# Three small VectorE operations of a routing step issued earlier and without a wait behind each

## The reference, cut to what matters

```python
def reference(**kwargs):
    attn_out = _attn_ref(...)                       # 4 x 8 heads, 768 positions, windowed attention
    x = attn_out.transpose(0, 2, 1, 3).reshape(3072, 512)
    x = _moe_ref(x=x, ...)                          # layer 0: 8 experts, each row goes to one
    return _moe2_ref(x=x, ...)                      # layer 1: 8 experts again, chosen anew

def _moe2_ref(x, expert_emb, tau, w1, w2):
    xn = x / (norm(x) + 1e-06)
    en = expert_emb / (norm(expert_emb) + 1e-06)
    logits = xn @ en.T / tau
    expert_idx = argmax(logits, axis=1)             # which expert of layer 1 gets the row
    ...
    out[mask] = gate_w[mask, None] * (relu(x[mask] @ w1[e]) @ w2[e])
```

## Time and profile before

| what | value |
|---|---|
| median of 3 runs | 1096.17 us |
| profiled execution, its own time | 1095.2 us |
| span of its instructions | 1093.6 us |
| PE, busy share of the span | 94% |
| DVE, busy share | 55% |
| ACT, busy share | 31% |
| POOL, busy share | 18% |
| mean granted TensorE clock | 0.980 of full speed |
| layer 0, from the first ranks to the last | 253 to 695 us |

### The profile page before, as it was taken

The page is one execution under the profiler, slowest core; times in us unless marked ns, Lnnn a source line. Parts: engine busy times, 40 slices in busy tenths (PEclk is TensorE's granted clock), DMA queues, the critical chain, the costliest instruction groups (busy, mean ns, idle before and its releaser), DMA issues.

```text
span 1093.6 us, 24687 instructions
## 1 busy us (share of the span) xinstructions
PE 1028.2 (94%) x6898; PEld 737.1 (67%) x6898; DVE 600.8 (55%) x2649; ACT 343.2 (31%) x1125; POOL 195.9 (18%) x390
## 2 busy tenths in 40 slices
PE   5999999989989999999999998999999999999994
PEld 4788888876756657675767664776667676675772
DVE  6678888855495676566656566433343334333331
ACT  4667766734132232222222222112122112121111
POOL 1022222221131222122222112211111111111111
PEclk9999999999999999999999999999999999999997
DMA  9965557663133514151415152514615153311110
GB/s 176 214 155 138 145 135 222 261 246 113 35 103 127 187 49 174 40 185 48 175 40 187 36 189 69 178 49 151 229 39 192 40 192 113 122 32 44 39 33 19
DMA packets 123518, 134.65 MB, mean 123 GB/s; under 512 B 82220, under 2 KB 82220, under 8 KB 123312
## 3 DMA queue, kind: packets, MB, share of 16 engines
q1 hardware_dynamic: 92672, 53.06, 19.2%
q10 hardware_dynamic: 23104, 59.11, 15.0%
q0 software_dynamic: 7664, 21.56, 5.5%
HBM read 105.55 MB, written 26.92 MB: 121 GB/s over the span
## 4 chain that ended last, share of the span: by engine, by line
PE 56%; issue 23%; DMA 9%; POOL 4%; DVE 4%; POOLq 1%; ACT 1%; ACTq 1%; DVEq 0%; SPq 0%
PE bank L1520 15%; PE bank L1530 14%; PE bank L1418 9%; DMA bins<-q_in,sidx 9%; PE bank L1460 5%; PE bank L1499 4%; PE bank L1646 3%; PE bank L1625 3%; POOL q_in L827 3%; PE bank L1434 2%; POOL pad_p L770 2%; ACT h_t L999 0%; DMA n_words<-in_n_local_dram 0%; POOLq L852 0%; DMA x_g<-bins 0%
## 5 line engine op out<-in xcount | busy, mean ns | idle before, releaser
L1520 PE MATMUL bank<-x_gt,w_sb 128*128 128x128 f32 x1856 | 219.0, 280 | 7.0 <-issue 7.0
L1520 PEld LDWEIGHTS bank<-x_gt,w_sb 128*128 128x128 f32 x1856 | 215.0, 195 | 15.5 <-issue 15.5
L1530 PE MATMUL bank<-w_sb,h_t 128*128 128x512 f32 x464 | 208.1, 601 | 3.2 <-DVE y_two L1328 2.6
L770 POOL TENSOR_TENSOR pad_p<-zeros 128x1 f32<-128x1 f32 x159 | 37.2, 234 | 824.7 <-DVE sidx L1344 240.5
L1530 PEld LDWEIGHTS bank<-w_sb,h_t 128*128 128x128 f32 x464 | 87.2, 193 | 102.0 <-issue 99.2
L986 ACT ACTIVATE h_t<-bank 128x256 f32<-128x256 f32 x168 | 63.2, 382 | 279.8 <-PE bank L1520 274.5
L1520 PE MATMUL bank<-x_gt,kv 128*128 128x128 f32 x832 | 98.3, 280 | 6.3 <-ACTq L1038 3.7
L1520 PEld LDWEIGHTS bank<-x_gt,kv 128*128 128x128 f32 x832 | 96.8, 196 | 10.5 <-issue 10.5
L1530 PE MATMUL bank<-kv,h_t 128*128 128x512 f32 x208 | 91.7, 593 | 0.0
L1323 DVE CAST sidx<-r 128x1 int32<-128x1 f32 x31 | 4.8, 154 | 147.6 <-PE bank L1530 117.3
L1351 DVE CUSTOM_DVE_ANT_0 k_t<-y_two,nbias 128x512 f32<-128x512 f32 x128 | 80.8, 686 | 0.0
(11 more groups left out here) (205 smaller groups left out, 1447.3 us busy)
## 6 DMA issues: line engine op xcount, KB each, us to landing
w_sb<-in_moe_w_dram ACTq DMA_DIRECT2D x18, 2048.0 KB, 13.8
kv<-in_moe_w_dram ACTq DMA_DIRECT2D x8, 2048.0 KB, 11.7
x_g<-bins SPq DMA_DIRECT2D x120, 133.0 KB, 2.7
w_sb<-in_moe_w_dram SPq DMA_DIRECT2D x4, 2048.0 KB, 13.2
q_in<-in_q_dram SPq DMA_DIRECT2D x24, 256.0 KB, 3.8
kv<-in_k_dram SPq DMA_DIRECT2D x24, 256.0 KB, 4.8
kv<-in_v_dram SPq DMA_DIRECT2D x24, 256.0 KB, 3.4
kv<-in_moe_w_dram SPq DMA_DIRECT2D x2, 2048.0 KB, 16.8
```

The lines of the kernel that those rows point to most:

```text
L770: return nc.gpsimd.tensor_tensor(pad_p[:, at:at + 1], zeros[:, 0:1], zeros[:, 0:1], ALU.add)
L1520: m_ = T.matmul(banks[k][:, f * P:(f + 1) * P], w1[:, c * FF + at:c * FF + at + P], x_gt[:, c, :], start=(c == 0), stop=(c == KC - 1))
L1530: m_ = T.matmul(banks[4][:, :], h_t[:, c, :], w2[:, c * DM:(c + 1) * DM], start=(c == 0), stop=(c == FC - 1))
```

## The change

Three instructions move, and the waits behind them go. `issue` is a new helper: it raises `L.link` as `chain` does, but lets the queue run on. The validity (line 1362) and the running sum (line 1363) now stand ahead of the eight dots, and the empty-row offset (line 1343) stands ahead of the wait for the ranks. The number of links in a slot stays 13.

```diff
+                def issue(ins):
                     nonlocal no
                     no += 1
                     ins.then_inc(L.link, 1)
+
+                def chain(ins):
+                    issue(ins)
                     dve.wait_ge(L.link, STEP_LINKS * at + no)
 ...
                 def y_rows(i):
 
+                    ids = pay[:, bass.ds(i, 1), 2 * E:2 * E + 1].rearrange("p o c -> p (o c)")
+                    issue(V.tensor_scalar(r1[:, 1:2], ids, 0.0, OFF, ALU.is_equal, ALU.mult))
                     dve.wait_ge(L.rank, i + 1)
-                    ids = pay[:, bass.ds(i, 1), 2 * E:2 * E + 1].rearrange("p o c -> p (o c)")
                     chain(V.tensor_tensor(cmp1[:, :], banks[6][:, 0:E], hot1[:, :], ALU.mult))
                     chain(V.tensor_reduce(r1[:, 0:1], cmp1[:, :], AX.X, ALU.add))
-                    chain(V.tensor_scalar(r1[:, 1:2], ids, 0.0, OFF, ALU.is_equal, ALU.mult))
                     V.tensor_tensor(sidx[:, :], r1[:, 0:1], r1[:, 1:2], ALU.add).then_inc(L.pos, 1)
 
                 def next_scores(i):
 
                     dve.wait_ge(L.y, i + (1 + FIRST))
                     V.memset(pad_v[:, 0:1], 0.0)
+                    ids = pay[:, bass.ds(i + 1, 1), 2 * E:2 * E + 1].rearrange("p o c -> p (o c)")
+                    issue(V.tensor_scalar(r1[:, 4:5], ids, 0.0, None, ALU.is_gt))
+                    issue(V.tensor_tensor(pre1[:, :], pre1[:, :], hot1[:, :], ALU.add))
                     for e in range(E):
 ...
-                    ids = pay[:, bass.ds(i + 1, 1), 2 * E:2 * E + 1].rearrange("p o c -> p (o c)")
 ...
                     chain(V.tensor_reduce(r1[:, 3:4], cmp1[:, :], AX.X, ALU.max))
-                    chain(V.tensor_scalar(r1[:, 4:5], ids, 0.0, None, ALU.is_gt))
-                    chain(V.tensor_tensor(pre1[:, :], pre1[:, :], hot1[:, :], ALU.add))
                     V.tensor_scalar(hot1[:, :], cmp1[:, :], r1[:, 3:4], r1[:, 4:5], ALU.is_equal, ALU.mult)\
```

More of the change, by code:

```diff
@@ L1273, in here @@
                     at, no = i, 0
-                def chain(ins):
+                def issue(ins):
                     nonlocal no
```

## The result

The changed kernel takes 1082.68 us, the median of 6 runs (1077.68 to 1084.12), against 1095.72 (1090.95 to 1097.47, 6 runs) before: a ratio of 0.9881, 95% interval 0.9853 to 0.9908.

The account below looks back on a forecast made before the run. The prediction took layer 0's half-tile path through the one-hot choice to bound the kernel; 2.28 + 2.85 + 0.26 + 1.01 = 6.40 us off 1095.2 gave 1088.8, from the median 1089.8, forecast 1089.0, range 1085.2 to 1092.4.

Parts of the forecast that it names:

- What bounds the kernel: Layer 0, half tiles: TensorE's waits for the one-hot choice (6.6 us) and gaps behind them (9.5 us) share one cause.
- Rival B: Loop-bound loads wait for the rank matmuls, not the choice; only the visible wait goes: 5.1 us, 1090.1 us; chance 0.11.
- c: Delay from validity and running sum put ahead of the dots: 0.25 us, bounds 0 to 0.51.
- Rival A: Instructions without a wait are no cheaper, so the delay ahead of the dots is 0.51: 1090.9 us; chance 0.13.
- The tail of the argmax and `y_rows`: Time removed by moving instructions out: 0.51 us behind the argmax, 0.31 us between the ranks and `sidx`.
- Single experts: Ends of experts with one half tile: choice 0.57 us earlier, four times, 2.28 us.
- Doubles: Ends of experts with two half tiles: 0.95 us earlier, three times, 2.85 us.
- The end: End of layer 0, through to the first product of layer 1: 1.01 us gained.
- The first looped tile: Gap at 270.13, where addresses are fixed: 0.26 us gained.
- The clock: TensorE's granted clock drops after some gaps; no term in the sum, forecast only set near the lower figure.
- rival C: Shorter gaps at ends of experts save one or two clock drops: 1085.5 to 1087.5 us; chance 0.13.
- rival D: Clock falls more often at ends of experts: 1090.3 to 1096 or more; chances 0.07 (one to four), 0.03 (five or more).

Follow-up runs that it names:

- g1: Changed kernel with TensorE's queue loading the next expert's two loop bounds between its full and half tiles; 1073.23 us, ratio 0.9802 to before.
- g2: Kernel before the change, with only the next expert's two loop bounds loaded earlier, between full and half tiles; 1078.11 us, ratio 0.9851.
- g3: Changed kernel's order, but each of the three moved instructions has its wait behind it again; 1088.10 us, ratio 0.9936 to before.
- the second pair: Kernel before and changed kernel, each measured and profiled once more without edits; 1095.79 and 1086.26 us.

## Why the prediction was wrong

The sign, and the path on which it rested, were right. Its terms against what was measured:

- *What bounds the kernel*: shown. The gap ahead of the next expert's product is the two loads (g1, g2) and a tail of the wait for the choice: the product follows the choice by 1.87 and 1.90. Rival B is out: the single experts gave the whole advance, not the visible 0.31.
- *Ahead of the dots*, c: 0.27 for 0.25. Rival A is out by g3.
- *The tail of the argmax and `y_rows`*: 0.51 and 0.31, as measured.
- *Single experts*: 0.68 to 0.75 each for 0.57. I had taken the copy's end as moving with the dots. It now lies inside them, and DVE waits for it 8 times and not 20. From y to line 1362 are 6.47 where 6.34 stood (625.47 to 631.81), so only 0.13 of the 0.25 put ahead of the dots counts. *Doubles*: 1.07 on average for 0.95, unevenly. *The end*: 1.15 for 1.01. *The first looped tile*: 0.21 for 0.26. The sum is 7.4 us for 6.4 in the two profiles, 7.3 in the second pair, and 5 to 7 by the clock-free times.
- *The clock*: this is the step that failed. The sum was made as if the time lost to it stayed, and rival C had "one or two" falls fewer, a chance of 0.13, and 1085.5 to 1087.5. Over all executions the remainder fell from 21.7 to 15.5 and 16.4 us, about as much as the path gave. The mistake was to price the falls from one profile, where three of seven ends had one, as an accident that might move either way ("which ones did not go by the length of the gap", under rival D), when the change shortens exactly the idle time that they follow. Every end lost 0.3 to 1.0 us of idle, and four of seven went below anything that was followed by a fall in any of the thirteen profiles. Half of seven ends at 1.6 us each is 5 to 6 us at stake. The range allowed for one fall fewer, and rival C for 1.5 to 3.5 us.
- *The scatter ahead of layer 0* was not in the prediction at all: the first ranks stood between 248.4 and 254.8 us over the thirteen profiles, with the same code ahead of them. One profile's span is worth no more than that. The first comparison of medians, 13.0, was partly luck: the second gave 9.4, and its 1086.26 us would have been inside the range without the step being any better.

The falls at the ends of experts explain some of the 5 to 6 us, not all: in the two pairs of profiles they cost 4.7 and 6.4 before and 3.3 and 3.3 after, some 2 us less. A further 1.7 us lies behind the wait for y in layer 1 (2.62 us of idle before, 2.40 after): over all profiles the clock fell there behind 2.58 to 2.62 us in four of four, and behind 2.39 to 2.43 us in five of nine. What decides it there, and what makes up the rest, stays open.

## What to carry to other kernels

A queue that stops at a wait also stops the register loads behind it, and they show up as a gap that names no engine: take the two as one, or move the loads ahead of the wait, which here took off at least as much as the change itself. When an edit shortens idle time of TensorE, list how long it is idle at each place before and after, and look at what the clock did behind each; a short wait can count twice where a fall would follow it. Between the small VectorE instructions here a wait cost 0.13 us each (steps of 0.20 and 0.07), and where they do not depend on each other the place for them is under a wait that stands anyway.

## What the runs showed of the hardware that was not expected

Amid dense matmuls the clock fell behind quite short idle times: in 24 of 38 cases between 1.36 and 2.49 us, and in none of 53 with 1.30 us or less. Behind the one wait for ScalarE ahead of the first looped tile it fell in none of nine, with 1.34 to 1.84 us. Which ends fall differs between two profiles of one kernel (412, 469 and 578 in the first of before; 318, 467, 520 and 577 in the second). The Trainium skill (TensorE: Matmul & The Clock Gate, What's actually happening) says something like it of a kernel's start: how many matmuls run slowly there differs from run to run of the same kernel. An unwaited step between two small instructions took 0.07 us and a waited one 0.20.
